# Five identity-by-identity products per attention unit on TensorE, written to PSUM banks that nobody reads

## The reference

```python
for t in range(S):
    new_re = ar * S_re - ai * S_im
    new_im = ar * S_im + ai * S_re
    S_re, S_im = (new_re + k[t] (x) v[t], new_im)
    y[t] = q[t] . S_re
x = y as (3072, 384)
x = sum over e of P[:, e] * (relu(x @ w1[e]) @ w2[e])
out = gate_w * (relu(x @ w1[own]) @ w2[own])
```

## Time and profile before

| | |
|---|---|
| median of 3 runs | 2676.65 us (2671.6 to 2677.28) |
| the profiled execution's own time | 2671.95 us |
| its span, first to last instruction | 2669.9 us |
| TensorE busy | 2485.4 us, 93% of the span, 14026 matmul instructions |
| VectorE, ScalarE, GpSimd busy | 43%, 28%, 7% |
| mean granted TensorE clock | 0.904 of full speed |

### The profile page before, as it was taken

How to read it: one execution, slowest core, us unless ns; L and a number is a source line. 1 busy time by engine, 2 the same in 40 slices (tenths; PEclk the granted TensorE clock), 3 DMA queues, 4 the chain that set the end, 5 groups by cost and what they waited for, 6 DMA issues and landing times. The chain is left out here.

```text
span 2669.9 us, 41004 instructions
## 1 busy us (share of the span) xinstructions
PE 2485.4 (93%) x14026; PEld 2368.0 (89%) x14027; DVE 1155.6 (43%) x2533; ACT 747.7 (28%) x1293; POOL 188.1 (7%) x176
## 2 busy tenths in 40 slices
PE   0498999999999999999999999999999999589998
PEld 0277877888999999999999999999999999578897
DVE  6876767533444333333333333333333332475533
ACT  4555555332211221211211211211211212154322
POOL 0000000000110110110110110110110100022221
PEclk9965555565999999999999999999999999699999
DMA  3102111110100000000000000000000001243210
GB/s 120 35 29 69 45 66 48 33 33 1 48 25 0 24 24 0 24 24 0 24 24 0 24 24 0 24 24 0 24 24 0 24 24 51 101 141 129 82 41 20
DMA packets 44715, 96.78 MB, mean 36 GB/s; under 512 B 4101, under 2 KB 26651, under 8 KB 44640
## 3 DMA queue, kind: packets, MB, share of 16 engines
q1 hardware_dynamic: 40672, 84.97, 9.2%
q0 software_dynamic: 3968, 10.82, 1.3%
HBM read 161.83 MB, written 10.81 MB: 65 GB/s over the span
## 5 line engine op out<-in xcount | busy, mean ns | idle before, releaser
L982 PE MATMUL bank<-x_parts,w_hi 128*128 (+1 forms) x3072 | 783.5, 335 | 0.1
L867 ACT ACTIVATE h_hi<-bank 128x384 fp32r<-128x384 f32 x512 | 250.1, 492 | 1250.2 <-PE bank L982 1250.1
L982 PEld LDWEIGHTS bank<-x_parts,w_hi 128*128 128x128 f32 x3072 | 554.3, 188 | 0.2 <-DVEq L904 0.2
L936 DVE SCALAR_TENSOR_TENSOR h_lo<-bank,h_hi 128x384 fp32r<-128x384 f32 x512 | 283.8, 557 | 577.1 <-ACT h_hi L867 577.1
L982 PE MATMUL bank<-x_parts,w_lo 128*128 (+1 forms) x1536 | 513.8, 335 | 0.0
L994 PE MATMUL bank<-w_hi,h_hi 128*128 128x384 f32 x1536 | 513.3, 334 | 0.0
L994 PE MATMUL bank<-w_hi,h_lo 128*128 128x384 f32 x1536 | 513.1, 334 | 0.0
L994 PE MATMUL bank<-w_lo,h_hi 128*128 128x384 f32 x1536 | 513.0, 334 | 0.0
L956 DVE SCALAR_TENSOR_TENSOR mixed<-bank,gate,mixed 128x384 f32 (+1 forms) x336 | 207.6, 618 | 442.7 <-PE bank L994 442.7
L982 PEld LDWEIGHTS bank<-x_parts,w_lo 128*128 128x128 f32 x1536 | 288.9, 188 | 0.0
L994 PEld LDWEIGHTS bank<-w_lo,h_hi 128*128 128x128 f32 x1536 | 288.3, 188 | 0.0
(11 more groups left out here) (197 smaller groups left out, 2229.1 us busy)
## 6 DMA issues: line engine op xcount, KB each, us to landing
routed_w_raw<-in_moe_w SPq DMA_DIRECT2D x64, 1536.0 KB, 6.6
w_raw<-in_moe_w SPq DMA_DIRECT2D x32, 768.0 KB, 6.0
q_k<-in_qk SPq DMA_DIRECT2D x24, 512.0 KB, 3.7
decay<-in_a SPq DMA_DIRECT2D x20, 528.0 KB, 5.0
v_rows<-in_v SPq DMA_DIRECT2D x24, 192.0 KB, 2.4
mixed_rows<-mixed SPq DMA_DIRECT2D x4, 1152.0 KB, 4.6
decay<-in_a SPq DMA_DIRECT2D x4, 432.0 KB, 4.9
routed_x<-mixed_rows,gather_now POOLq DMA_INDIRECT x31, 3.2
```

What stands on the lines that cost most here:

```text
L867: nc.scalar.activation(h_parts[par][0][:, c, :], h_bank[c], ACT.Relu).then_inc(h_hi, 1)
L936: nc.vector.scalar_tensor_tensor(out=h_parts[par][1][:, c, :], in0=h_bank[c], scalar=0.0, in1=h_parts[par][0][:, c, :].bitcast(F32), op0=A ...
L982: last = nc.tensor.matmul(h_bank[c].rearrange("p (u s) -> p u s", u=SUB), w1_parts[half][w][:, k, c * PT:(c + 1) * PT], mem.x[:, bass.ds(b ...
```

## The change

A helper `keep_warm(bank)` multiplies the identity (as the stationary operand) by the identity repeated four times (512 moving columns) and writes the 128 x 512 result to a whole bank. It is called once per unit that passes a state on, into `kt_re`, between `turn_x(u - 1)` and the output, and four times after the output of each unit but the last, into `sc_a`. No wait and no signal is added, and no other instruction moves.

```diff
--- before.py
+++ after.py
@@ -624,6 +624,10 @@
                     last = nc.tensor.matmul(square_sums, ident[:, :], sq[:, :, part, :], start=part == RE, stop=part == IM)
                 last.then_inc(summed, 1)
 
+            def keep_warm(bank):
+                nc.tensor.matmul(bank[:, :], ident[:, :], ident[:, :].unsqueeze(1).to_broadcast([PT, BANK // PT, PT]),
+                                 start=True, stop=True)
+
             sum_squares(0)
             pe.wait_ge(gate_w_split, 1)
             for u in range(UNITS):
@@ -678,6 +682,8 @@
 
                 if u:
                     turn_x(u - 1)
+                if passes_on(u):
+                    keep_warm(kt_re)
                 if c:
                     pe.wait_ge(wide_ready, kept(u))
                 if u >= 2:
@@ -694,6 +700,9 @@
                         last = nc.tensor.matmul(yb[:, h * D:(h + 1) * D], sc[:, h, :], vn[:, u % 3, h, :],
                                                 start=c == 0, stop=c == 0 or h % 2 == 1)
                 last.then_inc(y_done, 1)
+                if u + 1 < UNITS:
+                    for n in range(4):
+                        keep_warm(sc_a)
             turn_x(UNITS - 1)
             logits(UNITS - 2)
             logits(UNITS - 1)
```

## The result

The changed kernel took 2642.97 us (median of 4 runs, 2633.79 to 2650.26) against 2676.97 us for the kernel before in the same comparison. The ratio is 0.9876, with a 95% interval of 0.9857 to 0.9894. That is 34 us less; 36 were forecast.

What follows compares the result with a forecast made beforehand. TensorE at low clock and VectorE's and ScalarE's 14.7 us chain were taken to bound units together. Gains of 18 + 18 + 0 = 36 us off 2676.65 gave 2641 us, range 2592 to 2712, leaving out products that don't count.

Steps and rivals of the forecast that it cites:

- Two chains that end together: In one unit, TensorE's own work and VectorE's and ScalarE's 14.7 us chain end within 0.1 us at the squares.
- Products that count for the clock: The added products raise TensorE's clock by early in the output; windows of 160 to 660 us go from 0.57 to 0.8 or more.
- The rival that they don't: Added products on TensorE don't raise the clock and only cost time: 2857 us, chance 0.16.
- Their price: Each product is two instructions on TensorE, 0.43 us each at full clock, 0.85 at half.
- Units 4 to 16: Thirteen units held by the 14.7 us chain fall to 22.4 us each, gaining 1.4 x 13 = 18 us.
- the sign: Units 4 to 16 take 21 to 23 us, most with a new TensorE wait for ScalarE's squares.
- the shared part: Sum of squares, logits and odd scores, where both chains have joined: 9.0 us before, 6.3 at full clock.
- a quarter of 5.2: Charge of 1.3 us per unit in units 4 to 16 for clock lost between squares and odd scores.
- the floor of 21.1: Least time of units 4 to 16 with full clock from the squares on: 14.7 + 6.3 + 0.1 us.
- Units 17 to 22: Six units held by TensorE's own sum fall to 20.8 us each, gaining 3.0 x 6 = 18 us.
- The rest: Units 0 to 3 and 23, and the dense and routed stages: a gain of 0.
- The rival of idle time in front of the squares: Waiting for squares drops the clock: 17 us lost, 2694; decides above half of the heavy units; chance 0.12.

Runs made afterwards that it cites:

- e5: The kernel before, without any added product, with ScalarE's decays and squares of unit u + 2 placed ahead of its wait for the new state: 2669.4 us.
- e4: The changed kernel with ScalarE's decays and squares of unit u + 2 placed ahead of its wait for the new state, except a batch's first unit: 2610.5 us.
- e7: The changed kernel with each product of 512 columns replaced by eight transposes of the identity: 2643.1 us.
- e1: The changed kernel without the four products behind the output, keeping the one before it: 2669.5 us.
- e12: The changed kernel with two products behind the output instead of four, squares late as before: 2660.5 us.
- e3: The changed kernel with the four products moved from behind the output to just before the sum of squares: 2674.2 us.
- e6: e4 with two products behind the output instead of four: 2601.0 us.
- e9: e4 without the four products behind the output, keeping the one before it: 2621.6 us.

## Why the prediction was right

Point by point.

- **Two chains that end together.** Right, and shown by e5, e4 and the result together: either edit alone leaves a chain of about the old length in most heavy units (4 to 16). The squares land 14.7 us after the mask in all units from 0 to 15 but 4, 5, 10 and 11, before and after.
- **Products that count for the clock.** Right: the clock went from 0.57 to 0.84. The rival that they don't (0.16) was wrong, and so was the rule that stood behind it (e7).
- **Their price.** The eight take 3.67 us with the modelled tail, 0.44 each; 0.43 was forecast.
- **Units 4 to 16.** They took 294.2 us where they had taken 307.5: a gain of 13.3, against 18 forecast, 22.6 us per unit instead of 22.4; seven of the thirteen lie in the 21 to 23 us that were named as the sign. Of the 4.7 us missing, 1.6 had not been there to gain (the forecast started from 23.78 us in all thirteen; their mean was 23.66). The other 3.0 are in the end: the squares started 15.0 us after the mask on average, not 14.8, and the shared part took 7.6, just what the forecast had (6.3 and a quarter of 5.2). The mean of the shared part is right, its shape is not, and that is luck. It does not lose a bit in each unit:
  - five units kept the clock over the squares and took 21.1 to 21.6 us (7, 8, 9, 13, 15), around the floor of 21.1;
  - six lost it after a wait in front of them. Of these 6, 12 and 14 took 23.6 to 23.7, next to no gain. Units 4 and 10, before a batch's start, stayed at 25.2: there the squares wait for the scan of the decays and land 15.9 to 16.0 us after the mask, and the shared part took 9.24. Unit 16 took 20.9 (21.5 before), as the next unit passes no state on and so has no products of k and v between its odd scores;
  - units 5 and 11 gained nothing either (22.7 and 22.8). TensorE's unit 5 or 11 passes no state on, so it has no product before the output. The output ran at half clock, and the four behind it moved the squares from 13.7 to 15.1 and 15.5 us after the mask, which ate up what the shared part won (from 9.0 to 7.6 and 7.3).
- **Units 17 to 22.** 118.3 us instead of 133.9, a gain of 15.6 against 18 forecast. That this is close is luck in part. The forecast started from 23.8 us and ended at 20.8. The means were 22.3 (two of the six, 19 and 22, took 19.0 and 18.8 already) and 19.7: both ends were too high, by 1.5 and 1.1 us.
- **The rest.** The first four units gained 3.5 us, the second mask of unit 0 came 3.2 later, and 2.4 us came from behind the last second mask. In all 13.3 + 15.6 + 3.5 - 3.2 + 2.4 = 31.6 us, the difference of the two spans to within rounding (2669.9 and 2638.4). The 3.2 is not a price of the products, as none of them runs before that mask: in the other runs it came at 116.9 to 119.7 us. The zero for this part was 2.7 short, against some 7 that the two other terms had too much. So the profiled pair gained 4.5 less than forecast; the medians, with 34, are closer.
- **The rival of idle time in front of the squares** was given 0.12 as a whole. As a mechanism it is real, and its sign (a wait for squares, then squares at or near half clock) is there in six of the thirteen units. That is less than the half at which it was to decide, and it cost less than its price: no shared part took longer than the 9.24 us that units 4 and 10 had needed before. The price was paid elsewhere, in units of 25 to 26 us in e1 and e12. The forecast's own quarter of 5.2 us had the same event in it under another name: it was put down to logits and odd scores. But e3, where the shared part never took 9.0 us once products stood in front of the squares, shows that it was the wait ahead of them; what logits and odd scores themselves lose is at most the 1.2 us between 6.4 and 7.6 there.

The prediction missed one thing that did not show in its sum: that the four products fill the wait for VectorE's scale as well (e3).

## What to carry to other kernels

When an engine's clock depends on how busy it is, as TensorE's did here, an edit is judged by where its time is waited away afterwards. Work that filled a wait cost nothing and kept the clock for what followed; the same work where nothing is waited for was paid in full (units 17 to 22 of e6 against e9). Before adding it, find what the faster engine will wait for next: here moving ScalarE's squares ahead of an unrelated wait was worth 7 us alone and 34 on top of the products. And try the count on the chip: fewer products were 10 us better with early squares and 17 worse with late ones.

## What the runs showed of the hardware

- In the changed kernel each of eight waits of 2.0 to 4.6 us in front of the squares was followed by squares of 3.4 to 3.8 us, and behind none or up to 0.95 us of waiting they took 1.98. The clock was seen to fall inside the wait (unit 10: 1.00 up to 360.9, 0.50 from 361.1, the squares start at 361.80).
- The length of the wait alone does not decide. The kernel before waited 2.22 us at 578.14 and kept its clock, and so did unit 1 of e12 after 2.50:

```profile
156.86 1.98 PE L624 MATMUL bank<-squares,ident 128*128 128x512 f32 x4 [2.50 <-ACT squares L523]
```

- Float32 transposes of the identity lift the clock like float32 products of the same streaming time (2643.1 and 2643.0 us, 0.84 in both).
- The time does not follow the amount of added work: 2601, 2618 and 2610.5 us for two, three and four products behind the output, the last two not told apart. Why is open.
